# Gate folded into the output products, dense low parts on GpSimd, and a reordered beginning, in a fused delta-rule and two-MoE kernel

## What is computed

```python
k_n = k / (norm(k) + 1e-6)
for t in range(S):                                   # delta rule, one 48x48 state per batch and head
    y[:, :, t] = einsum('bhd,bhde->bhe', q[:, :, t], state)
    v_old = einsum('bhde,bhd->bhe', state, k_n[:, :, t])
    state += beta[t] * einsum('bhd,bhe->bhde', k_n[:, :, t], v[:, :, t] - v_old)
x = y as 3072 x 384
x = ((x @ w_a) * (x @ w_b)) @ w_out                  # w_a, w_b 384x1536, w_out 1536x384
logits = x @ w_gate + modality_bias[modality_id]     # 8 experts
e_idx = argmax(logits); gate = softmax(logits)[e_idx]
for e in range(8):                                   # w1 384x1024, w2 1024x384 per expert
    out[mask] = gate[mask] * (relu(x[mask] @ w1[e]) @ w2[e])
```

## Time and profile before

| | |
|---|---|
| runs | 1084.71, 1084.55, 1078.48 us (median 1084.55) |
| profiled execution, own time | 1078.09 us |
| its span, first to last instruction | 1076.3 us |
| mean granted TensorE clock | 0.941 |
| busy: PE, PE weight loads, DVE, ACT, GpSimd | 954.2, 825.6, 505.1, 297.3, 322.5 us |
| DMA | 170.12 MB, mean 158 GB/s |

### The profile page before, as it was taken

How to read it: one execution, slowest core, us unless ns; L and a number is a source line. 1 busy time by engine, 2 the same in 40 slices (tenths; PEclk the granted TensorE clock), 3 DMA queues, 4 the chain that set the end, 5 groups by cost and what they waited for, 6 DMA issues and landing times.

```text
span 1076.3 us, 27301 instructions
## 1 busy us (share of the span) xinstructions
PE 954.2 (89%) x10964; PEld 825.6 (77%) x10965; DVE 505.1 (47%) x1098; ACT 297.3 (28%) x552; POOL 322.5 (30%) x589
## 2 busy tenths in 40 slices
PE   2354999999999998999999999999946999999995
PEld 2343788888788877888888888888845999999995
DVE  3865655466546655566446653333373222222221
ACT  3022223233322232323233333232311222222221
POOL 1112133334233323434333434332401222222221
PEclk8656999999999999999999999999966999999998
DMA  8494357856675576655765565443538611171110
GB/s 251 159 217 153 106 166 226 228 165 192 175 213 171 179 211 179 199 177 182 207 178 179 164 181 163 153 151 114 162 106 258 205 44 44 44 264 50 37 44 24
DMA packets 150649, 170.12 MB, mean 158 GB/s; under 512 B 109567, under 2 KB 115841, under 8 KB 150544
## 3 DMA queue, kind: packets, MB, share of 16 engines
q0 software_dynamic: 32800, 114.65, 32.1%
q1 hardware_dynamic: 117744, 53.94, 20.1%
HBM read 99.34 MB, written 69.40 MB: 157 GB/s over the span
## 4 chain that ended last, share of the span: by engine, by line
PE 76%; DVE 11%; DMA 7%; issue 3%; ACT 2%; POOL 1%; SPq 0%; DVEq 0%; POOLq 0%; ACTq 0%
PE bank L508 19%; PE bank L510 18%; PE bank L509 18%; DMA work<-we_in 3%; PE bank L554 2%; DVE work L981 2%; PE bank L468 2%; PE bank L684 2%; PE bank L478 2%; PE bank L454 2%; DVE work L985 2%; PE bank L498 2%; PE bank L420 2%; PE bank L488 1%; PE bank L577 1%
## 5 line engine op out<-in xcount | busy, mean ns | idle before, releaser
L508 PE MATMUL bank<-wbuf,x_hi 128*128 128x512 f32 (+1 forms) x582 | 245.7, 422 | 3.5 <-DVE x_lo L1308 2.3
L510 PE MATMUL bank<-wbuf,x_lo 128*128 128x512 f32 (+1 forms) x582 | 230.5, 396 | 0.0
L509 PE MATMUL bank<-wbuf,x_hi 128*128 128x512 f32 (+1 forms) x582 | 230.1, 395 | 0.0
L739 ACT ACTIVATE work<-bank 128x512 f32<-128x512 f32 (+1 forms) x193 | 105.0, 544 | 351.8 <-PE bank L510 198.6
L1377 POOL DMA_DIRECT2D expert_split_scratch<-work x128 | 70.0, 547 | 418.6 <-DVE work L1029 405.2
L508 PE MATMUL bank<-wbuf,g_hi 128*128 128x384 f32 (+1 forms) x488 | 172.5, 353 | 5.2 <-issue 2.6
L510 PE MATMUL bank<-wbuf,g_lo 128*128 128x384 f32 (+1 forms) x488 | 164.2, 336 | 0.0
L509 PE MATMUL bank<-wbuf,g_hi 128*128 128x384 f32 (+1 forms) x488 | 163.9, 336 | 0.0
L1029 DVE TENSOR_TENSOR work<-work 128x384 fp32r<-128x384 f32 x128 | 71.0, 555 | 145.1 <-ACT work L739 144.8
L508 PEld LDWEIGHTS bank<-wbuf,x_hi 128*128 128x128 f32 x582 | 111.1, 191 | 27.4 <-issue 2.9
L510 PEld LDWEIGHTS bank<-wbuf,x_lo 128*128 128x128 f32 x582 | 110.8, 190 | 25.9
(11 more groups left out here) (143 smaller groups left out, 1242.2 us busy)
## 6 DMA issues: line engine op xcount, KB each, us to landing
expert_split_scratch<-work POOLq DMA_DIRECT2D x256, 192.0 KB, 3.2
work<-we_in POOLq DMA_DIRECT2D x128, 192.0 KB, 3.6
work<-a_in POOLq DMA_DIRECT2D x24, 896.0 KB, 6.9
wbuf<-expert_split_scratch SPq DMA_DIRECT2D x24, 768.0 KB, 5.8
work<-wm_in POOLq DMA_DIRECT2D x18, 384.0 KB, 5.5
inverse_in_scratch<-work SPq DMA_DIRECT2D x24, 256.0 KB, 2.8
work<-a_in SPq DMA_DIRECT2D x6, 768.0 KB, 6.1
x_scratch<-work SPq DMA_DIRECT2D x48, 96.0 KB, 2.5
```

The source lines that it names most:

```text
L508: pe.matmul(o, a_hi, w_hi, start=first, stop=False)
L509: pe.matmul(o, a_hi, w_lo, start=False, stop=False)
L510: return pe.matmul(o, a_lo, w_hi, start=False, stop=last)
L739: return act.activation(o, i, ACT.Copy)
```

## The change

Five things are changed.

1. **Gate.** w_out is multiplied by w_gate once, at the start: `gate_products` on PE, from a transposed copy of w_out (`wt_in`) that GpSimd's queue loads in 6 parts of 768 columns ahead of the dense pieces. The 12x8 columns of the result are split in high and low parts (`gate_hi`, `gate_lo`) and stand behind each block of w_out in `wbuf`. `out_products` is then 392 columns wide instead of 384 and gives the logits too. `y_transposes`, `logits`, ACT's `y_t` and their semaphores are gone.
2. **Buffers.** Raw dense weights have six buffers (`RING`), three where they were and three new ones.
3. **Low parts.** All 18 dense low parts are made by GpSimd. The first 12 stand directly behind `triangle(0)` and `v_scale(0)`, each with the load of a later piece behind it; 12 to 17 stand in slot 0. ACT makes high parts 3 to 11 before slot 0, 12 and 13 behind `u_copy(0)`, 14 to 17 behind `x_split(0)`.
4. **Order.** GpSimd's first load waits for the third `kk_products`. SyncE's queue loads the small tensors and the constants before the first `store_at`. `at_form(4)` to `(8)` and the norms of group 2 are placed anew, and group 1's chain stands in slots 1 and 2 (`FIRST_SUB`) instead of 0 to 2. In a slot with norms, `norm_sum` stands behind `s_add` instead of ahead of `w_form`.
5. **Bank.** `x_transposes` writes bank 4 instead of bank 6, waits for `a_copy` instead of the last `g_split`, and stands ahead of `out_products(t, 1)`.

```diff
-WM = 2 * KD * FF + (FF // P) * D
+OUT_W = D + E
+WM = 2 * KD * FF + (FF // P) * OUT_W
 WB_AT, WO_AT = KD * FF, 2 * KD * FF
...
+RING = 6
+PARTS = 6
...
+        def staged(q):
+            r = q % RING
+            if r < 3:
+                return work[:, raw_at + r * SPLIT1:raw_at + (r + 1) * SPLIT1]
+            return a_raw[:, r - 3, :]
...
-            for n in range(GROUP):
-                store_at(n)
-            load_tb(0)
-            load_kt_pair(4)
-            load_kt_pair(6)
-            load_ke(1)
-            load_t12(0)
-            load_t12(1)
-            sp.dma_start(cst[:, :], const_in).then_inc(S["const"], 16)
-            load_kt(8)
-            store_inverse(0)
-            for n in range(GROUP):
-                load_hh(n)
...
             sp.dma_start(b_wg, wg_in).then_inc(S["small"], 16)
...
             sp.dma_start(b_mid[:, 0, :].bitcast(I32), mid_in.bitcast(I32)).then_inc(S["small"], 16)
+            sp.dma_start(cst[:, :], const_in).then_inc(S["const"], 16)
+            for n in range(GROUP):
+                store_at(n)
+            load_tb(0)
+            load_t12(0)
+            load_ke(1)
+            load_kt_pair(4)
+            load_kt_pair(6)
+            load_t12(1)
+            store_inverse(0)
+            for n in range(GROUP):
+                load_hh(n)
+            load_kt(8)
+            load_ke(2)
...
                 else:
-                    pe.wait_ge(S["gl"], NF * t)
+                    pe.wait_ge(S["acp"], NF * t)
                 for k in range(KD):
-                    mm = pe.transpose(bank[6][:, k * P:(k + 1) * P], a_y[:, p, k * P:(k + 1) * P], ident)
+                    mm = pe.transpose(bank[4][:, k * P:(k + 1) * P], a_y[:, p, k * P:(k + 1) * P], ident)
                 mm.then_inc(S["xtr"], 1)
...
                 if t == 0:
-                    pe.wait_ge(S["lo"], (6, 12, 12)[n])
+                    pe.wait_ge(S["dlo"], (3, 9, 9)[n])
...
             def b_products(t, n):
                 m = t * NF + n
+                if t == 0:
+                    pe.wait_ge(S["dlo"], (6, 12, 12)[n])
...
                 pe.wait_ge(S["gm"], m + 1)
-                if n == 0 and t >= 1:
-                    pe.wait_ge(S["lsb"], t)
-                elif n >= 1:
+                if m >= 1:
...
                 if t == 0 and n == 0:
-                    pe.wait_ge(S["lo"], ND)
+                    pe.wait_ge(S["dlo"], ND)
+                if t == 0 and n == 0:
+                    pe.wait_ge(S["wgl"], 1)
...
                 for k in range(4):
-                    w = WO_AT + (4 * n + k) * D
-                    mm = split_matmul(bank[7][:, 0:D], g_hi[:, m % 2, k * P:(k + 1) * P],
-                                      g_lo[:, m % 2, k * P:(k + 1) * P], wbuf[:, w:w + D],
-                                      wbuf[:, WM + w:WM + w + D], n == 0 and k == 0,
+                    w = WO_AT + (4 * n + k) * OUT_W
+                    mm = split_matmul(bank[7][:, 0:OUT_W], g_hi[:, m % 2, k * P:(k + 1) * P],
+                                      g_lo[:, m % 2, k * P:(k + 1) * P], wbuf[:, w:w + OUT_W],
+                                      wbuf[:, WM + w:WM + w + OUT_W], n == 0 and k == 0,
...
+            def gate_products(i):
+                pe.wait_ge(s_rd[i], 16)
+                for j in range(2):
+                    o = gate_sums[:, (2 * i + j) * E:(2 * i + j + 1) * E]
+                    for k in range(KD):
+                        w = staged(i)[:, (j * KD + k) * P:(j * KD + k + 1) * P]
+                        mm = pe.matmul(o, w, b_wg[:, k, :], start=(k == 0), stop=(k == KD - 1))
+                mm.then_inc(S["wgm"], 1)
...
-                if b1:
-                    y_transposes(t - 1)
...
-                if b1:
-                    logits(t - 1)
...
                     g_transposes(t, 2)
-                    out_products(t, 1)
                 if a:
                     x_transposes(n)
                 if b:
+                    out_products(t, 1)
...
-            for n in range(AHEAD):
+            for n in range(GROUP):
+                kk_products(n)
+            pe.wait_ge(S["small"], 48)
+            for i in range(PARTS):
+                gate_products(i)
+            for n in range(GROUP, AHEAD):
...
-            def y_t(t):
-                act.wait_ge(S["ytr"], t + 1)
-                copy(b_yT[:, 0, :], bank[6][:, 0:D]).then_inc(S["yt"], 1)
+            def gate_hi():
+                act.wait_ge(S["wgm"], PARTS)
+                copy(gate_piece(0), gate_sums.rearrange("p (b w) -> p b w", w=E)).then_inc(S["wgh"], 1)
...
             sqrt(0)
-            for i in range(6):
+            for i in range(3):
                 hi_dense(i)
+            gate_hi()
             square(1)
+            for i in range(3, 12):
+                hi_dense(i)
             sqrt(1)
-            hi_dense(6)
...
+            def gate_lo():
+                dve.wait_ge(S["wgh"], 1)
+                dve.tensor_tensor(gate_piece(1), gate_sums.rearrange("p (b w) -> p b w", w=E),
+                                  gate_piece(0).bitcast(F32), ALU.subtract).then_inc(S["wgl"], 1)
...
             def take_logits(t):
-                dve.wait_ge(S["lg"], t + 1)
-                dve.tensor_copy(b_logit[:, t, :], bank[6][:, D:D + E]).then_inc(S["lsb"], 1)
+                dve.wait_ge(S["y2sb"], t + 1)
+                dve.tensor_copy(b_logit[:, t, :], bank[7][:, D:OUT_W]).then_inc(S["lsb"], 1)
...
+            FIRST_SUB = {1: {MIDDLE: (1, 5), NEXT: (5, 8), LATE: (8, 13)},
+                         2: {EARLY: (13, 17), MIDDLE: (17, 21), NEXT: (21, 24), LATE: (24, 31)}}
...
-                if norm < GROUPS:
-                    norm_sum(norm)
-                    norm_guard(norm)
                 if a:
                     w_form(n)
...
+                if norm < GROUPS:
+                    norm_sum(norm)
+                    norm_guard(norm)
+                if b:
+                    g_split(t, 0)
+                if n == 1:
                     norm_sum(2)
                     norm_guard(2)
-                    lo_dense(6)
-                    lo_dense(7)
-                if b:
-                    g_split(t, 0)
...
-            for i in range(4):
-                lo_dense(i)
...
-            lo_dense(4)
-            lo_dense(5)
+            gate_lo()
             norm_root(1)
+            at_form(4)
+            at_form(5)
...
+            def load_part(q):
+                if q >= RING + PARTS:
+                    pool.wait_ge(S["dlo"], q - RING - PARTS + 1)
+                elif q >= RING:
+                    pool.wait_ge(S["wgm"], q - RING + 1)
+                src = wt_in[:, q * SPLIT1:(q + 1) * SPLIT1] if q < PARTS else wm_in[:, dense_columns(q - PARTS)]
+                pool.dma_start(staged(q), src).then_inc(s_rd[q % RING], 16)
+
+            def lo_dense(i):
+                pool.wait_ge(S["hi"], i + 1)
+                pool.tensor_tensor(dense_piece(i, 1), staged(PARTS + i).rearrange("p (b w) -> p b w", w=D),
+                                   dense_piece(i, 0).bitcast(F32), ALU.subtract).then_inc(S["dlo"], 1)
...
+                if n == 0:
+                    lo_dense(12)
+                    lo_dense(13)
...
+                    for i in range(14, ND):
+                        lo_dense(i)
+                    triangle(1)
...
+            pool.wait_ge(S["kk"], 3)
+            for q in range(RING + 3):
+                load_part(q)
             load_row(0)
-            load_dense(3)
-            load_dense(4)
+            for q in range(RING + 3, 2 * RING):
+                load_part(q)
             triangle(0)
-            load_dense(5)
-            load_dense(6)
             v_scale(0)
-            load_row(1)
-            load_dense(7)
-            load_dense(8)
+            for i in range(12):
+                lo_dense(i)
+                load_part(PARTS + RING + i)
+                if i == 5:
+                    load_row(1)
             v_scale(1)
```

More of the change, by code:

```diff
@@ L165, in kk_bank @@
         def kk_bank(n):
-            return bank[(0, 3, 4, 5, 6, 7, 3, 4)[n] if n < 8 else 3]
+            return bank[(0, 3, 4, 5, 6, 3, 4, 5)[n] if n < 8 else 3]
         r_m = rb.take(1, TILES)
@@ L216, in build @@
         s_row = [S["row0"], S["row1"]]
-        s_rd = [S["rd0"], S["rd1"], S["rd2"]]
+        s_rd = [S[f"rd{i}"] for i in range(RING)]
         s_raw = [S["raw0"], S["raw1"]]
@@ L638, in _ @@
                 slot(n)
-            y_transposes(TILES - 1)
-            logits(TILES - 1)
             pe.wait_ge(S["rpe"], 1)
@@ L853, in slot @@
                 if n == 0:
-                    for i in range(9, 12):
+                    for i in range(14, ND):
                         hi_dense(i)
@@ L1068, in sub_part @@
                 first, last = SUB.get(n % GROUP, {}).get(when, (1, 1))
-                if n == 0:
-                    first, last = {LATE: (1, 7)}.get(when, (1, 1))
-                if n == 1 and when == EARLY:
-                    first, last = 7, 12
```

(9 more changed lines are left out.)

137 lines of the change are left out of this document (49 added, 88 removed).

## The result

The changed kernel takes 1068.53 us (median of 4 runs, 1063.19 to 1070.86), the kernel before 1081.91 (4 runs, 1078.48 to 1084.71). The ratio is 0.9879, with a 95% interval of 0.9853 to 0.9906: faster by 1.2%, where 1052 us and a range of 1034 to 1068 were forecast. The profiled span is 1065.1 us instead of 1076.3.

What follows compares the result with a forecast made beforehand. PE's work was taken to bound steady slots, DVE's substitution and the buffers' round trip the beginning. Terms summed to -27.55, taking 1078.09 to 1050.5 us (1057 from the median run); forecast 1052, between the two, range 1034 to 1068.

Steps and rivals of the forecast that it cites:

- The start of the substitution: Beginning: group 0's substitution on DVE was to start at 27.5 us instead of 28.46, bounds 26 and 31.
- a faster keys' load: Beginning: with no weights beside the keys' load, the keys' products were to start 1 to 2 us sooner.
- The substitution: Group 0's chain on DVE: 23.1 us, plus 22.8 for twelve stalls of 1.90, plus 0.95 for `v_scale(1)`.
- From the chain to the dense products, and slot 1: Substitution's end to first dense products: 19.8 us instead of 23.7; then slot 1 at 32.8, slot 2 starting 1.0 later.
- The 22 slots: Slots 2 to 23: -18.0 us of PE work, -3.6 of `g_lo` waits, -3.9 and -1.4 at norms, +0.7 in slot 2.
- PE's work in a slot: Steady slots: no `y_transposes` or `logits`, but wider output products; 0.82 us less a slot, -18.0 over 22 slots.
- The waits for `g_lo`: PE's 12 waits ahead of `x_transposes`, 9.1 us: the moved transposes give 0.30 us more work before each; -3.6, bounds 0 and -9.
- The norms: Slots 3, 7 and 11: shorter waits for `w_form` give -3.9 us, and less time at half clock -1.4.
- The tail: End of the kernel: the logits' copy follows the copy of y at once, -2.05 us; routing and experts untouched.
- The last slot: Its end is paced by expert pieces with a round trip through HBM, so it gives only -0.3 us.
- that of half the steady gain given back: Rival: DVE's or ACT's order bounds the steady slots; 9 us lost there, norm waits of 5 stay; 1066 us, chance 0.15.
- That the low parts come too late for the lock: Rival: no lock under the substitution, DVE's chain ends near 51, 22.8 + 0.95 us more won; 1028 us, chance 0.10.

Runs made afterwards that it cites:

- `loads_behind_blocks`: The changed kernel with group 0's triangle first on GpSimd's queue and all its loads behind it; 1049.99 us, ratio 0.9697.
- `three_parts`: The changed kernel with the triangle behind three of w_out's six parts on GpSimd's queue, all other loads behind it; 1062.22 us, ratio 0.9839.
- `tri_early`: The changed kernel with the triangle behind w_out's six parts and ahead of the six loads that wait for gate products; 1062.54 us, ratio 0.9825.
- `low_behind_chain`: The changed kernel with GpSimd's low parts 0 to 11 made only after group 0's substitution has ended; 1063.95 us, ratio 0.9851.
- `loads_and_low_moved`: The changed kernel with the triangle ahead of all GpSimd's loads and low parts 0 to 11 on DVE, behind the substitution; 1044.19 us, ratio 0.9658.
- `norms_back`: The changed kernel with `norm_sum` and its guard ahead of `w_form` again in slots 3, 7 and 11; 1073.71 us, ratio 0.9926.

## Why the prediction was wrong

The direction held, the time was 16.5 us off. By its own terms, the span of 1065.1 us against the 1048.7 that its sum gave:

- **The start of the substitution: +10.2 us. This is the step that failed.** It was put at 27.5 with bounds 26 and 31; it came at 37.75. The prediction wrote that w_out's last part is issued near 15 us and lands ahead of the blocks' load. That is so, and it missed what matters: the blocks' load waits for the inverse's stores, and these run at the same time as w_out. `loads_behind_blocks`, `three_parts` and `tri_early` show it in steps: 7.3 us from 26.18 to 33.47 for six parts. It also named three loads that wait for PE, and gave them no price; there are six of them (parts 6 to 11; seven more loads stand ahead of the triangle, not six), 2.56 us apart, while PE makes the gate products at a granted clock of 0.50. The blocks' load, running beside them, landed 4.3 us later than in `tri_early`. 7.3 + 4.3 is the whole way from 26.18 to 37.75. The upper bound of 31 came from no row for either. Nor did the 1 us come that a faster keys' load was to win: the keys' products started at 7.16 us instead of 9.26, but DVE scales them behind the norms, at 11.36 (before: 11.28).
- **The substitution: right, with two small errors that cancel.** 46.32 us for 46.85. The stretch by the low parts is 46.32 - 22.88 (`low_behind_chain`) = 23.4, over 12: 1.95 us each for 1.90. The low part itself takes 1.82 us, not 1.68, and the stall is 1.07 times it, not 1.13. The Trainium skill's rule (SBUF — State Buffer, Who interferes with whom) is that two SBUF inputs on DVE meet GpSimd's reads in one exclusive lock. The trace agrees with it: 12 x 1.82 = 21.9 by it, 23.4 measured.
- **From the chain to the dense products, and slot 1: right.** 19.66 for 19.8, and 33.3 for 32.8. In slot 1 the first stretch at half pace, for which no run shows the seven us of the prediction, was shorter: the granted clock was 0.50 from 103.73 to 108.20, 4.5 us, and 0.94 on average behind it; the waits were 3.2 us for 2.7. So the sum is nearer than its terms, by luck. The 24.3 us that `loads_and_low_moved` wins are a price of the new beginning, nearly twice the 13.4 us by which the change made the kernel faster.
- **The 22 slots: +5.9.** 616.85 instead of 637.20 us is 20.35 less; 26.2 was predicted. Two terms were mis-sized. *PE's work in a slot* fell by 0.64 us, not by 0.82: the products of 392 columns take about 0.2 us more per slot, not 0.13 (0.178 us from start to start instead of 0.173), and leaving out `logits` gives 0.55, not 0.65, since the last dense product's end (0.10 us) is now waited out by the across product. 22 x 0.18 = 4.0. (The prediction says that it keeps 2 us for the wide products; its sum doesn't hold them.) *The waits for `g_lo`* around the transposes were to fall by 3.6. At `x_transposes`, now at the output products, they fell from 9.1 to 6.1, but ahead of `g_transposes` they grew from 1.8 to 3.4: 1.4 won, 2.2 missed. The prediction treated them as a cover of 0.30 us each and did not ask what made `g_lo` late. At the longest, 2.33 us, it was an expert row that landed late, which the order of PE doesn't move; how much of the rest is that is not shown.
- **The norms: right.** Slots 3, 7 and 11 took 8.0 us less in sum, 3 x 0.64 of it the work that every slot lost. That leaves 6.1; 5.3 was predicted, and `norms_back` gives 5.2, with the wide interval said there.
- **The tail: right.** 288.90 for 291.00 us, and the logits' copy 0.1 us behind ACT's: -2.1 for -2.05. The last slot gave nothing instead of 0.3. The terms add up to 10.2 - 0.5 - 0.1 + 0.5 + 5.9 + 0.4 = 16.4, the whole difference.

Of the rivals, that of half the steady gain given back named the measured time (1066), with 9 us lost in the slots and 5 behind the norms. It was not that: the slots lost 6, the norms nothing, and the beginning 10. That the low parts come too late for the lock (1028) came true in `loads_behind_blocks`, by moving the loads; of what it gave, a part was lost behind the chain, where the later weights wait for the low parts.

## What to carry to other kernels

Before a load is moved ahead, list which transfers on the critical path are in flight at that moment, also those of other queues, and count the bytes put beside them; that the new load itself lands in time says nothing of them. A load that waits for a consumer (here PE at half clock) holds everything behind it on its queue, here the triangle until 33.93, a bound hidden only by the later landing at 36.27; so a short operation of the critical chain belongs ahead of such loads. And work handed from DVE to GpSimd beside a chain of DVE operations on SBUF can cost the chain more than twice what it would cost on DVE: compare the stall with DVE's own time for it first.

## What the runs showed of the hardware

- Stores in small packets are delayed by loads in big packets on another queue, by each load alike: 1.0 to 1.2 us for each of up to six loads of 384 KB beside four stores of 256 KB, which land in 3.5 us alone (`loads_behind_blocks`) and in 8.7 beside w_out. The Trainium skill (DMA: Bandwidth & Descriptors, Queues, rings and completion order) says that a DMA engine takes turns between its queues, a whole packet at a time. The row agrees as far as it goes: both queues moved in the same 13 us, and the weights' 564 packets, most of them of 6 KB, took 60.9% of the engines' time, the other queue's 4160 packets of some 250 bytes 34.9%. Whether the skill's packet is the one that the profile counts, and what another size of packet would do, no run here shows.
- GpSimd's subtraction of 768 columns takes 1.82 us against DVE's 0.95, 1.9 times; the prediction put it at twice the 0.84 us of 384 columns, and it is a little more.
- The lock reaches small operations too: in `loads_behind_blocks` a DVE operation of 32 columns on SBUF took 2.04 us beside a low part, and 0.19 in `loads_and_low_moved`, where GpSimd had none there. An operation with one input in PSUM took its usual 0.56 us beside one in the changed kernel (at 103.80).
